# Score matmuls in PE tiles of 64 rows by 32 columns

## The chip, the cores and the metric

The kernel runs on one core of a Trainium2 chip. The metric is the device time of one execution in microseconds; lower is better. Three executions were timed before the change, and one more was recorded by the hardware profiler.

## What is computed

Three stages follow each other. The first is a linear attention with decay over 4 batches, 8 heads, 768 tokens and 48 features a head:

```python
for t in range(S):
    cur = np.einsum('bhd,bhe->bhde', u[None] * kt, vt)
    y[:, :, t] = np.einsum('bhd,bhde->bhe', rt, state + cur)
    state = w[None, :, :, None] * state + np.einsum('bhd,bhe->bhde', kt, vt)
```

The second and the third are `g(x @ w_in) @ w_out` over the 3072 tokens with 384 features and 2048 hidden units; the second has a leaky ReLU with a slope for each hidden unit, the third has `h * tanh(softplus(h))`.

## The kernel before, in words

**Work items.** The tokens are cut into 24 chunks of 128 tokens (a batch has six) and into 8 tiles of 384 tokens, three chunks each. The 8 heads of a chunk make four pairs. A unit is one pair of one chunk, so there are 96 units, numbered w = 4c + p. Head q of a pair (0 or 1) has its 48 features in partitions 64q to 64q+47, so that it takes one half of TensorE's rows.

**Scores by levels.** The 128x128 lower triangle of scores of a chunk is not computed at once, because the decay between two tokens must be split between a scaled key and a scaled query. It is cut into seven levels. Level l has m = 2^l: in every block of 2m tokens, the second m tokens (queries) look at the first m (keys). GpSimd scales the keys and queries of levels 1 to 6 (L272, L262); level 0 takes the rows as they came. `score` (from L993) writes for each level the products of all 128 keys with the 64 tokens that are queries at this level, head q into PSUM bank q, keys on partitions, at the columns `level_columns(l)`. What isn't needed of this is never read: ScalarE copies the blocks of the high levels (`copy_high`, L804), VectorE picks the low ones under a mask (`pick_scores`, L539). So keys of one half only meet queries of their half: two halves of 64 keys, each with 32 queries, two heads, four matmuls for each of levels 0 to 5; level 6 has the first 64 keys alone, against 64 queries, two matmuls. That is 26 matmuls (L1021) a unit. They are float32, and the profile shows each as two pairs of a weight load and a matmul: 52 pairs a unit. Keys are the stationary operand, queries the moving one.

**A unit on the engines.** ScalarE writes the diagonal of the scores (`fill_diagonal`, L792), waits for the unit's score matmuls, and copies the high levels (L804). VectorE then adds the chunk's sum into the running state (`advance_state`, L523), which waits for these copies, and picks the low levels (L539, five instructions). TensorE then runs `attend`: the state's part (L1038) and, after the picks, scores times values (L1043). Before the scores of a unit TensorE computes the chunk's sum of keys times values (L1005).

**Order on TensorE.** In the first tile units run alone (`first_tile`). Then `tile1` runs 16 steps for each tile, and in each step: the up projection of the tile before (`up`, L960, nine matmuls of 384 columns), `attend` of the unit of the last step, `score` of this step's unit, and the down projection of two steps back (`down`, L976, nine matmuls). Of 16 steps 12 have a unit. Meanwhile ScalarE has for each step the two ReLU parts (L841, L842) and the high part of the hidden values (L771), and VectorE the activation (L636) and their low part (L618), each in a fixed order with the unit's work between them. The third stage (`tile2`) has no units.

The lines that the change and the working touch: L1015 to L1021 in `score`, and the readers L804, L523 and L539.

Of the kernel before, what the change touches and what calls it, by code (L numbers as in the profile page):

```python
# [39 lines left out]
CHUNK = 128  # L40
CHUNKS = TOKENS // CHUNK
PAIRS = H // 2
HALF = 64
ROWS = HALF + D
LEVELS = CHUNK.bit_length() - 1
LOW = 5
# [23 lines left out]
def spread(ap, axis, n):  # L70

    wide = ap.unsqueeze(axis)
    return wide.broadcast_to([n if i == axis else k for i, k in enumerate(wide.shape)])


def build(nc, rk_t, rkv, decay, bonus, slope, weights, out):
# [4 lines left out]
    with ctx:  # L81
        def sb(name, shape, dt=F32):
            return ctx.enter_context(nc.sbuf_tensor(name, shape, dt))

        def sem(name):
# [21 lines left out]
                                                                l=LEVELS - 1)  # L107
# [19 lines left out]
        half = sb("half", [P, 1])  # L127
# [11 lines left out]
        hid2 = hid + [lev[:, i] for i in range(2)]  # L139
        U0 = (LEVELS - 1) * HALF  # L140


        rev_table = acc[0][:, 0:PAIRS * HALF].rearrange("p (a t) -> p a t", a=PAIRS)
        fwd_table = acc[2][:, 0:PAIRS * HALF].rearrange("p (a t) -> p a t", a=PAIRS)

# [57 lines left out]
        block = ctx.enter_context(nc.Block())  # L203
# [28 lines left out]
        def level_banks(rep, p):  # L232

            return hid_pair if rep == 0 and p % 2 else lev

        def level_columns(l):

            first = (l - 1) * HALF if l else U0 + D
            return slice(first, first + HALF)

# [14 lines left out]
        def scale_query_level(engine, par, x, l, early):  # L255

            pairs = slice(2 * x, 2 * x + 2)
            m = 1 << l
            src = rk_rows[0:ROWS, par, 0, pairs].rearrange("p a (i b m) -> p a i b m", b=2, m=m)[:, :, :, 1]
            dst = queries[0:ROWS, x, l - 1].rearrange("p (a i m) -> p a i m", a=2, m=m)  # L260
            table = fwd_table if early else power
            return engine.tensor_tensor(dst, src, spread(table[0:ROWS, pairs, 0:m], 2, CHUNK // (2 * m)), ALU.mult)  # L262


        def scale_key_level(engine, par, x, l, early):

            pairs = slice(2 * x, 2 * x + 2)
            m = 1 << l
            src = rk_rows[0:ROWS, par, 1, pairs].rearrange("p a (i b m) -> p a i b m", b=2, m=m)[:, :, :, 0]
            dst = keys[0:ROWS, x, l - 1].rearrange("p (a i b m) -> p a i b m", a=2, b=2, m=m)[:, :, :, 0]  # L270
            table = rev_table if early else power_rev[:, :, CHUNK - HALF:CHUNK]
            return engine.tensor_tensor(dst, src, spread(table[0:ROWS, pairs, HALF - m:HALF], 2,  # L272
                                                         CHUNK // (2 * m)), ALU.mult)
# [663 lines left out]
        def _(pe):  # L937
# [45 lines left out]
            def ready(c, w, p, rep):  # L983

                if rep == 0:
                    reached(pe, mask_done, w - 1)
                elif p == 0:
                    pe.wait_ge(mask_done, w)
                if p % 2 == 0:
                    pe.wait_ge(key_done, 2 * c + p // 2 + 1)  # L990
                    pe.wait_ge(q_done[p // 2], c + 1)

            def score(c, w, par, p, rep, ends):  # L993


                x = p // 2
                banks = level_banks(rep, p)
                if not ends:
                    ready(c, w, p, rep)
                    if p == 0:  # L1000
                        pe.wait_ge(kstate_done, c + 1)
                    for q in range(2):
                        rows = slice(HALF * q, HALF * (q + 1))
                        h = 2 * p + q
                        nc.tensor.matmul(banks[rows, 0, U0:U0 + D], k_state[:, p, rows],  # L1005
                                         rkv_tok[:, par, 2, D * h:D * (h + 1)], start=True, stop=True)

                for l in reversed(range(LEVELS)):
                    if l:
                        k = keys[:, x, l - 1].rearrange("p (a t) -> p a t", a=2)[:, p % 2]  # L1010
                        t = queries[:, x, l - 1].rearrange("p (a t) -> p a t", a=2)[:, p % 2]
                    else:
                        k = rk_rows[:, par, 1, p]
                        t = rk_rows[:, par, 0, p].rearrange("p (i b) -> p i b", b=2)[:, :, 1]
                    parts = 1 if l == LEVELS - 1 else 2  # L1015
                    for half in range(parts):
                        tokens = slice(HALF * half, HALF * (half + 1))
                        wanted = slice(HALF // parts * half, HALF // parts * (half + 1))
                        for q in range(2):
                            rows = slice(HALF * q, HALF * q + D)  # L1020
                            last = nc.tensor.matmul(banks[tokens, q, level_columns(l)][:, wanted], k[rows, tokens],  # L1021
                                                    t[rows, wanted], start=True, stop=True)
                last.then_inc(score_done, 1)
# [23 lines left out]
            def first_tile():  # L1047

                units = CHUNKS_PER_TILE * PAIRS
                pe.wait_ge(zero_act, 3)  # L1050
                for w in range(units):
                    c, p = divmod(w, PAIRS)
                    score(c, w, c % 2, p, 0, False)
                    if w > 0:
                        c, p = divmod(w - 1, PAIRS)
                        attend(c, w - 1, c % 2, p, 0, c == 0)
                c = CHUNKS_PER_TILE - 1
                attend(c, units - 1, c % 2, PAIRS - 1, 0, False)
                score(c + 1, units, (c + 1) % 2, 0, 1, False)

            def tile1(t, rep):
                odd = rep % 2
                for j in range(STEPS):
                    s = STEPS * (t - 1) + j
                    if rep > 1 or j >= 2:
                        pe.wait_ge(glo_done, s - 1)
                    now = unit_at(j) if rep < TILES and (rep < TILES - 1 or j + 1 < STEPS) else None
                    if now:
                        c = CHUNKS_PER_TILE * t + now[0]
                        unit = (c, 4 * c + now[1], (odd + now[0]) % 2, now[1], rep)  # L1070
                    ends = now and odd == 1 and now[0] == CHUNKS_PER_TILE - 1
                    if ends and now[1] == 0:
                        ready(unit[0], unit[1], 0, rep)
                    up(s, j, 1 - odd, j + 1 if rep == 1 else None, hid[j % 2],
                       per_chunk * CHUNKS_PER_TILE * t if j == 0 else None)
                    if ends and now[1] == 2:
                        ready(unit[0], unit[1], 2, rep)
                    u = unit_at(j - 1)
                    if rep < TILES and u:
                        c = CHUNKS_PER_TILE * t + u[0]  # L1080
                        attend(c, 4 * c + u[1], (odd + u[0]) % 2, u[1], rep, odd == 0 and u[0] == 0)
                    if now:
                        score(*unit, ends)
                    if rep > 1 or j >= LAG1:
                        down((t - 1) if j >= LAG1 else (t - 2), (j - LAG1) % STEPS, ghi_done, s - LAG1 + 1,
                             glo_done, s - LAG1 + 1)
# [81 lines left out]
```

## Time and profile before

| what | us |
|---|---|
| runs (three) | 1051.43, 1058.20, 1057.89 |
| median | 1057.89 |
| the profiled execution | 1052.23 |
| its span, first to last instruction | 1050.2 |
| first tile, units alone | about 0 to 75 |
| tiles with units in their steps | about 75 to 580 |
| the rest, without units | 580 to 1050 |

The span is 2 us shorter than the time of the same execution; a change of the span counts one for one. PE stands for matmuls, PEld for weight loads. Durations of matmuls are modelled and overlap, so that their starts tell more than their ends. A row of the windows view counts the instructions that touch a stretch, with their busy time as a union.

### The profile page before, as it was taken

What the parts mean: (1) busy time and instruction counts of PE and PEld (TensorE: products, weight loads), DVE (VectorE), ACT (ScalarE), POOL (GpSimd) and SP (SyncE); (2) the same over time, 40 slices, a digit from 0 to 9 for tenths busy, and PEclk for the clock granted to TensorE, in tenths of its full rate; (3) what the DMA queues carried; (4) which work ended last, traced back from release to release, by engine and by line L of the source; (5) the groups of instructions that cost most, each with busy time, mean ns of one, the idle gap of its engine ahead of it and who ended that gap; (6) DMA issues with size and microseconds to landing.
All of it is one profiled execution on the core that took longest, in us unless ns stands there. A gap on an engine that the chain in (4) does not pass through costs nothing.

```text
span 1050.2 us, 28000 instructions
## 1 busy us (share of the span) xinstructions
PE 1001.7 (95%) x10628; PEld 949.2 (90%) x10628; DVE 692.5 (66%) x1643; ACT 684.7 (65%) x1698; POOL 378.2 (36%) x674
## 2 busy tenths in 40 slices
PE   4668999999989999999999999999999999999998
PEld 3557889999889999899999999999999999999998
DVE  6458676656646655566566444877777777787875
ACT  6545655455544555555555567888888888888885
POOL 7556657656646655556563062000000000000000
PEclk9999999999999999999999999999999999999999
DMA  3223322112121221221120243100000000000000
GB/s 107 88 77 118 118 73 66 43 43 66 44 68 44 58 66 46 58 70 49 43 66 6 103 120 98 61 24 24 24 23 22 22 22 22 22 0 22 1 23 23
DMA packets 22036, 54.50 MB, mean 52 GB/s; under 512 B 4640, under 2 KB 9376, under 8 KB 21920
## 3 DMA queue, kind: packets, MB, share of 16 engines
q1 hardware_dynamic: 19472, 43.43, 14.0%
q10 hardware_dynamic: 2448, 9.49, 2.3%
q8 instruction: 78, 1.28, 0.5%
q14 instruction: 38, 0.31, 0.1%
HBM read 41.10 MB, written 9.44 MB: 48 GB/s over the span
## 4 chain that ended last, share of the span: by engine, by line
PE 80%; ACT 4%; DVE 4%; issue 2%; DMA 2%; SPq 0%; ACTq 0%; DVEq 0%
PE acc L976 36%; PE hid L960 25%; PE lev L960 8%; PE lev L1021 7%; PE tok L1038 2%; PE tok L1043 2%; DMA w_raw<-weights 2%; DVE scores L539 1%; ACT scratch L884 1%; ACT scratch L885 1%; PE lev L1005 1%; DVE scratch L687 1%; ACT scores L792 0%; DVE scratch L680 0%; ACT scores L804 0%
## 5 line engine op out<-in xcount | busy, mean ns | idle before, releaser
L960 PE MATMUL hid<-x_parts,w_hi 128*128 128x384 f32 x1152 | 326.6, 337 | 9.5 <-DMA x_parts<-y 5.6
L976 PE MATMUL acc<-g_hi,w_hi 128*128 128x384 f32 x768 | 269.8, 351 | 1.6 <-ACT result L781 1.6
L976 PE MATMUL acc<-g_hi,w_lo 128*128 128x384 f32 x768 | 257.7, 335 | 0.0
L960 PEld LDWEIGHTS hid<-x_parts,w_hi 128*128 128x128 f32 x1152 | 212.6, 189 | 10.4 <-issue 10.2
L960 PE MATMUL hid<-x_parts,w_lo 128*128 128x384 f32 x576 | 194.0, 337 | 0.0
L841 ACT ACTIVATE relu_neg<-hid 128x384 f32<-128x384 f32 x128 | 62.6, 489 | 200.2 <-PE hid L960 199.7
L976 PE MATMUL acc<-g_lo,w_hi 128*128 128x384 f32 x768 | 175.1, 335 | 0.0
L539 DVE COPY_PREDICATED scores<-mask,lev 128x128 f32<-128x128 int8 x444 | 158.9, 358 | 12.0 <-issue 0.2
L636 DVE SCALAR_TENSOR_TENSOR hid<-relu_neg,neg_slope,hid 128x384 f32<-128x384 f32 x128 | 79.6, 622 | 128.3 <-ACT hid L842 128.2
L976 PEld LDWEIGHTS acc<-g_hi,w_hi 128*128 128x128 f32 x768 | 144.2, 188 | 11.1 <-issue 3.9
L272 POOL TENSOR_TENSOR scratch<-rk_rows,power_rev 112x128 f32<-112x128 f32 x240 | 97.4, 441 | 153.7 <-PE lev L1021 153.7
L976 PEld LDWEIGHTS acc<-g_hi,w_lo 128*128 128x128 f32 x768 | 144.6, 188 | 0.0
L976 PEld LDWEIGHTS acc<-g_lo,w_hi 128*128 128x128 f32 x768 | 137.2, 188 | 0.6 <-DVE g_lo L705 0.6
L262 POOL TENSOR_TENSOR scratch<-rk_rows,power 112x128 f32<-112x128 f32 x282 | 117.8, 454 | 0.1
L960 PEld LDWEIGHTS hid<-x_parts,w_lo 128*128 128x128 f32 x576 | 109.2, 190 | 0.0
L960 PE MATMUL lev<-x_parts,w_hi 128*128 128x384 f32 x384 | 107.6, 334 | 0.0
L891 ACT ACTIVATE scratch<-scratch,three_halves 128x384 f32<-128x384 f32 x128 | 78.7, 615 | 41.3 <-DVE scratch L687 40.8
L693 DVE SCALAR_TENSOR_TENSOR scratch<-scratch 128x384 f32<-128x384 f32 x128 | 71.5, 558 | 40.1 <-ACT scratch L891 40.1
L1021 PE MATMUL lev<-scratch 48*64 48x32 f32 (+1 forms) x3960 | 84.8, 229 | 0.0
L680 DVE TENSOR_SCALAR scratch<-scratch 128x384 f32<-128x384 f32 x128 | 46.1, 360 | 55.6 <-ACT scratch L885 55.6
L1021 PEld LDWEIGHTS lev<-scratch 48*64 48x64 f32 x3960 | 74.7, 141 | 7.5 <-issue 3.2
L618 DVE TENSOR_TENSOR g_lo<-hid,g_hi 128x384 fp32r<-128x384 f32 x128 | 70.6, 552 | 14.5 <-ACT g_hi L771 14.5
(95 smaller groups left out, 1534.1 us busy)
## 6 DMA issues: line engine op xcount, KB each, us to landing
rkv_tok<-rkv SPq DMA_DIRECT2D x24, 576.0 KB, 3.9
w_raw<-weights SPq DMA_DIRECT2D x32, 384.0 KB, 3.1
rk_rows<-rk_t SPq DMA_DIRECT2D x48, 192.0 KB, 3.3
x_dram<-result ACTq DMA_DIRECT2D x8, 576.0 KB, 3.1
rkv_tok<-x_dram SPq DMA_DIRECT2D x8, 576.0 KB, 3.7
out<-result ACTq DMA_DIRECT2D x8, 576.0 KB, 2.8
x_parts<-y SPq DMA_DIRECT2D x141, 16.0 KB
bonus_tok<-bonus SPq DMA_DIRECT2D x1, 192.0 KB, 5.5
```

The lines of the kernel that those rows point to most:

```text
L262: return engine.tensor_tensor(dst, src, spread(table[0:ROWS, pairs, 0:m], 2, CHUNK // (2 * m)), ALU.mult)
L272: return engine.tensor_tensor(dst, src, spread(table[0:ROWS, pairs, HALF - m:HALF], 2, CHUNK // (2 * m)), ALU.mult)
L539: nc.vector.copy_predicated(dst, pick, src).then_inc(pick_done if l < low_levels(rep) - 1 else mask_done, 1)
L618: nc.vector.tensor_tensor(g_lo[:, j % RING], hid[j % 2][:, 0:TILE], g_hi[:, j % RING].bitcast(F32), ALU.subtract).then_inc(glo_done, 1)
L636: nc.vector.scalar_tensor_tensor(hid[j % 2][:, 0:TILE], relu_neg[:, j % 2], neg_slope[:, j:j + 1], hid[j % 2][:, 0:TILE], ALU.mult, ALU.ad ...
L680: nc.vector.tensor_scalar(seed[:, d], seed[:, d], SEED_B, SEED_A, ALU.mult, ALU.add).then_inc(seed_done, 1)
L693: nc.vector.scalar_tensor_tensor(root[:, d], eps[:, d], 0.75, seed[:, d], ALU.add, ALU.mult).then_inc(root_done, 1)
L841: nc.scalar.activation(relu_neg[:, j % 2], hid[j % 2][:, 0:TILE], ACT.Relu, scale=-1.0)
L891: nc.scalar.activation(eps[:, d], eps[:, d], ACT.Square, scale=-1.0, bias=three_halves[:]).then_inc(sq_done, 1)
L960: last = nc.tensor.matmul(to[:, 0:TILE], w[:, j, kt * P:(kt + 1) * P], x[:, par, kt], start=x is x_hi and w is w_hi and kt == 0, stop=x is ...
L976: last = nc.tensor.matmul(acc[d][:, 0:TILE], w[:, j, cols], g[:, j % RING], start=j == 0 and g is g_hi and w is w_hi, stop=j == STEPS - 1 ...
L1021: last = nc.tensor.matmul(banks[tokens, q, level_columns(l)][:, wanted], k[rows, tokens], t[rows, wanted], start=True, stop=True)
```

## The change

`score` cuts the keys into groups of 32 instead of 64. With `block = max(2m, 32)`, a group of keys whose tokens are no keys at this level (second half of a block of 64 or 128) is left out, and a group meets only the queries of its own block. Levels 0 to 4 get four groups of 32 keys with 16 queries each, level 5 two groups with 32 queries, level 6 two groups with 64 queries; each for two heads. The outputs start at partitions 0, 32, 64 and 96, so that the eight combinations of head and key group take eight places of 64 rows by 32 columns. What is read later is the same.

```diff
+QUARTER = 32
...
-                    parts = 1 if l == LEVELS - 1 else 2
-                    for half in range(parts):
-                        tokens = slice(HALF * half, HALF * (half + 1))
-                        wanted = slice(HALF // parts * half, HALF // parts * (half + 1))
+                    m = 1 << l
+                    block = max(2 * m, QUARTER)
+                    for first in range(0, CHUNK, QUARTER):
+                        if first % block >= m > QUARTER // 2:
+                            continue
+                        tokens = slice(first, first + QUARTER)
+                        begin = first // block * block // 2
+                        wanted = slice(begin, begin + block // 2)
                         for q in range(2):
                             rows = slice(HALF * q, HALF * q + D)
                             last = nc.tensor.matmul(banks[tokens, q, level_columns(l)][:, wanted], k[rows, tokens],
```

## Rows read from the trace of the kernel before

**Rows 1.** The page: TensorE's share, its slices, and the chain that ended last.
```profile
PE 1001.7 (95%) x10628; PEld 949.2 (90%) x10628; DVE 692.5 (66%) x1643; ACT 684.7 (65%) x1698; POOL 378.2 (36%) x674
...
PE   4668999999989999999999999999999999999998
...
PE 80%; ACT 4%; DVE 4%; issue 2%; DMA 2%; SPq 0%; ACTq 0%; DVEq 0%
```

**Rows 2.** The windows view of L1021 alone: busy time and instructions by stage.
```profile
0.00:75.00 75.00, 23.46 (x723) 21.71 (x726) 1.00 0.34 95
75.00:138.00 63.00, 9.99 (x522) 8.88 (x520) 0.97 0.35 105
138.00:580.00 442.00, 72.80 (x3772) 64.72 (x3765) 1.00 0.18 53
```

**Rows 3.** Windows, L1021: one unit's burst, from its first load to the next line's.
```profile
308.47:309.41 0.94, 0.94 (x52) 0.89 (x52) 1.00 0.00 0
...
26.07:27.71 1.64, 1.64 (x52) 1.57 (x52) 1.00 0.45 125
```

**Rows 4.** Windows of 10 ns, L1021: matmuls, then loads, that touch each.
```profile
308.46:308.47 0.01, 0.00 (x0) 0.00 (x0) 1.00 0.00 0
...
308.50:308.51 0.01, 0.01 (x4) 0.01 (x4) 1.00 0.00 0
308.51:308.52 0.01, 0.01 (x4) 0.01 (x4) 1.00 0.00 0
308.52:308.53 0.01, 0.01 (x4) 0.01 (x5) 1.00 0.00 0
...
308.98:308.99 0.01, 0.01 (x16) 0.01 (x8) 1.00 0.00 0
309.00:309.01 0.01, 0.01 (x16) 0.01 (x12) 1.00 0.00 0
...
309.06:309.07 0.01, 0.01 (x16) 0.01 (x12) 1.00 0.00 0
```

**Rows 5.** Timeline of the loads after a burst: start, us, what.
```profile
304.66 0.19 PEld L976 LDWEIGHTS acc<-g_hi,w_hi 128*128 128x128 f32 x1
304.77 0.19 PEld L976 LDWEIGHTS acc<-g_hi,w_lo 128*128 128x128 f32 x1
```

**Rows 6.** Timeline of one step with the first unit of a chunk.
```profile
344.95 0.77 PEld L1021 LDWEIGHTS lev<-scratch 48*64 48x64 f32 x43
...
345.61 0.68 ACT L792 ACTIVATE scores<-ident,diag 128x128 f32<-128x128 f32 x2
...
346.37 0.61 ACT L804 ACTIVATE scores<-lev 64x128 f32<-64x128 f32 x3
...
347.35 1.91 DVE L539 COPY_PREDICATED scores<-mask,lev 128x128 f32<-128x128 int8 x5
...
349.21 0.17 PEld L1038 LDWEIGHTS tok<-r_state,state 112*48 112x48 f32 x4 [0.25 <-issue]
...
349.37 0.24 PEld L1043 LDWEIGHTS tok<-scores,rkv_tok 128*48 128x48 f32 x4
```

**Rows 7.** Timeline: later units of a chunk, the step after it.
```profile
327.71 0.61 ACT L804 ACTIVATE scores<-lev 64x128 f32<-64x128 f32 x3 [0.45 <-PE lev L1021]
...
328.69 1.93 DVE L539 COPY_PREDICATED scores<-mask,lev 128x128 f32<-128x128 int8 x5
...
331.05 0.24 PEld L1043 LDWEIGHTS tok<-scores,rkv_tok 128*48 128x48 f32 x4
...
332.67 0.61 ACT L804 ACTIVATE scores<-lev 64x128 f32<-64x128 f32 x3 [0.18 <-PE lev L1021]
```

**Rows 8.** Waits of PE, PEld and POOL for others: us in total, times, longest.
```profile
POOL scratch L272 <- PE lev L1021: 153.7, 20, 13.8
...
PEld tok L1043 <- DVE scores L539: 18.2, 25, 2.5
...
PE tok L1043 <- DVE scores L539: 11.8, 13, 2.1
```

**Rows 9.** Timeline of two units of the first tile: TensorE alone.
```profile
26.07 1.39 PE L1021 MATMUL lev<-scratch 48*64 48x64 f32 x42
...
28.33 0.67 PE L1043 MATMUL tok<-scores,rkv_tok 128*48 128x128 f32 x4 [0.55 <-DVE scores L539]
```

## The prediction

> **What bounds the kernel now.** I read the page first: how busy each engine is, the span in 40 slices, and the chain of work that ended last. TensorE is busy 95% of the span, its slices stand at 9 tenths (once 8) from the fifth on, and 80% of the last chain is TensorE's [rows 1]. So in most of the kernel a microsecond less on TensorE is a microsecond less of time, if nothing else is late next. The windows view of the changed line by stage shows how much there is to win: 73 us of the 442 between 138 and 580 us, 10 before that, and 23 in the first tile, where TensorE is not the bound; the last 470 us have no scores [rows 2]. Then I looked at one unit closely. From its first load to the first load of the down projection behind it a burst takes 0.94 us for 52 pairs of load and matmul, in the first tile 1.64 us [rows 3].
>
> **What sets a burst's 0.94 us.** There are four places in use (two heads by two key halves). The 10 ns windows show the rhythm. At the start the loads touching a window go from none to four within 40 ns: the four places are filled one after another, though in program order nine other pairs stand between the first pair and the one that opens the fourth place. A fifth load comes 50 to 60 ns after the first. Later the number of loads swings between 8 and 12, and 12 comes back about 60 ns later: four loads start nearly together, then nothing starts, then four again [rows 4]. So the engine doesn't run out of instructions; each place takes some 58 ns a pass. A pass of levels 0 to 5 streams only 32 columns. Its 58 ns are then mostly those of the load of 64 columns, in time for the next pass only. For a size that isn't 64 columns there is one pair of rows: the first load of 128 columns after a burst is followed by the next after 0.11 us [rows 5]. 64 columns in 55 ns and 128 in 110 ns make a load's time proportional to its columns.
>
> The sum fits. The places of the first key half have 14 passes (2 for each of seven levels), so 14 x 58 = 0.81 us, and 0.13 us is left for filling and draining: 0.94 us.
>
> **The change part by part.** *Instructions.* Levels 0 to 4 now have 8 matmuls each, levels 5 and 6 have 4 each: 48 matmuls, 96 pairs a unit in place of 52. Over 96 units that is 4224 more pairs. *Columns.* The loads fall from 52 x 64 to 96 x 32 columns, about the same in sum (3328 to 3072), but spread over eight places. *The longest place.* The places of keys 0 to 31 still have 14 passes, the others 12 or 10. Level 6 streams 64 columns as before; its two passes stay at 58 ns each, as a stream of 64 columns is about as long as its load was (estimate from attend's 128 columns, which come in about 0.11 us apart). The twelve others load 32 columns: half of 55 ns, plus the 3 ns by which 58 is over 55, about 31 ns. Their stream (16 columns, or 32 at level 5) fits into that. 2 x 58 + 12 x 31 = 0.49 us, plus 0.13 us for filling and draining: 0.62 us. Saved: 0.32 us a unit; I take 0.31, since eight places need 7 ns each to be filled.
>
> *Bounds of a pass.* No row has a 32-column load or eight places. From above: all 58 ns are fixed or shared, and nothing is won (0 us). In the middle: half is fixed (the matmul of a pass starts some 28 ns after its load) and only the other 27 ns halve, so 45 ns a pass, 2 x 58 + 12 x 45 = 0.66, and 0.79 us a unit: 0.15 saved. From below: a pass of 25 ns would save 0.39. Below nothing: if the engine could not start pairs faster than it does now on average (0.94/52 = 18 ns, or 0.79/52 = 15 ns without filling and draining), a unit would take 96 x 15 ns + 0.15 = 1.6 us, 0.67 us more. I take 31 ns, since the two load sizes seen lie on one line and the fill of the places at 7 ns each shows faster starts than 15 ns.
>
> The Trainium skill, TensorEngine Tiling (Array Packing), section Performance Considerations, speaks against this change: each matmul costs about 60 cycles whatever its free size, so one should not take a tiling factor from a dimension that is already small. Here the moving side shrinks from 32 to 16 columns. At 2.4 GHz that is 25 ns, and counted over the whole engine 96 x 25 ns = 2.4 us a unit. The trace doesn't agree with it in that sense, as 52 x 25 ns = 1.3 us is more than the 0.94 us measured; counted for each place it is under the 31 ns above.
>
> **What of it reaches the end.** *Steps with a unit, 138 to 580 us* (72 units). The mask of a unit must be there when the next step's attend starts. In the later units of a chunk ScalarE's copies wait for the scores (idle 0.45 and 0.18 us before L804 [rows 7]), so an earlier burst brings the mask earlier too; the picks end at 330.62 and attend's load starts at 331.05, 0.43 us spare. These units keep nearly all of the 0.31 us. In the first unit of a chunk no attend stands before the scores, and L804 starts right when L792 is done (345.61 + 0.68 against 346.37), about 0.45 us after the burst's end: ScalarE is the limit, and an earlier burst changes nothing for the mask. The picks end at 349.26, L1043 starts at 349.37 [rows 6]. With 0.31 us less before it, TensorE would wait 0.2 us there. That is so in about 13 of the 18 chunks, 2.4 us in all. The first unit of each tile already waits for VectorE (the view of waits has 25 waits of L1043's loads for L539, 18 us in sum [rows 8]); I leave about 7 units out. (72 - 7) x 0.31 - 2.4 = 17.8 us.
>
> *75 to 138 us* (some 10 units): here ScalarE and VectorE also split weights and TensorE often waits for the masks. Half of 0.31 for each: 1.5 us.
>
> *First tile* (12 units). A unit's attend waits for the picks (0.55 us idle [rows 9]), and the next score burst stands behind it; so the chain runs score, copies, picks, attend and the score of two units later, and a shorter burst counts once in two units. Matmuls are slower here, 1.64 us a burst [rows 3]. In the same proportion the saving is 0.31 x 1.64/0.94 = 0.54 us; twelve times, halved, 3.2 us. As DMA waits and VectorE's own work hold some of these units, I take 2.2.
>
> *At nothing.* GpSimd waits for scores, not the other way about, with 154 us of such waits [rows 8], and takes earlier keys gladly. VectorE at 66% and ScalarE at 65% [rows 1] are no bound on average. The reads of the scores don't change. Fetching 8448 more instructions has room, as a step of 4.9 us now has some 160 of TensorE's and would have 250; if that cover failed, it would be the slower case below.
>
> The sum: 17.8 + 1.5 + 2.2 = 21.5 us. From the profiled 1052.2 us that gives 1030.7. This execution lies 5.7 us under the median of the runs, 1057.9, near the lowest; from the median it would be 1036. I say 1033.
>
> **The rivals.** *A: half of a pass is fixed* (45 ns). 0.15 us a unit: mask waits are then small, 70 x 0.15 + 0.8 + 1.1, about 12 us; 1043. For it: the matmul of a pass starts 28 ns after its load. Against: the 128-column load would then be 83 ns and not 110.
> *B: places in the same rows share the path of the loads.* Four places of 32 columns need as long as two of 64, a pass stays at 58 ns, 14 of them: 1053 to 1058, no change. For it: the sum of columns stays, and two places by 27 ns would also give 55 ns. Against: four loads start within 20 ns and their next ones also, with none late. The same result follows if the masks turn out to hold TensorE everywhere: then only the first tile gains.
> *C, slower: starts become the bound.* One mechanism: pairs reach the array no faster than the 15 ns that the burst now shows. It decides from 0.81/96 = 8.5 ns a pair on; at 15 ns 0.67 us more for each of 84 units, with a mask that is spare longer: 56 us, 1108. At 10 ns it is 0.15 us a unit, 13 us, 1068. For it: no row shows more than a few starts at under 15 ns. Against: the fill at 7 ns a matmul, where at least ten pairs were at hand. The rule of the skill named above would give this sign.
> *D: the change doesn't do what it says*, for instance because the same drain and fill come between the groups of 32 as come between lines: that would be C again, in the profile as gaps inside a burst.
>
> **How the numbers follow.** My forecast (31 ns a pass, 28 to 36) 0.53; A 0.17; B 0.13; C with D 0.17. A measurement of this kernel can tell about 1% (10 us) from no change. Faster by over 1%: the forecast and all of A but the part close to the line, 0.69. Within 1%: B and that part, 0.14. Slower by over 1%: 0.17. The likeliest case's own range is 1025 to 1041. The 8 in 10 range reaches over A to the upper end of B, 1060; only C lies outside. The lower end, 1023, is a pass of 25 ns (0.39 us a unit: 27 us) from the profiled execution.
>
> **What would show it.** Right: L1021 with 96 pairs a unit and a burst of 0.62 us from its first load to the down projection's; eight loads together in the 10 ns windows every 31 ns or so; new waits of L1043 for L539 of about 0.2 us in the first unit of a chunk; the steps of later units at 4.6 instead of 4.9 us; 580 to the end unchanged at 470 us. Wrong: bursts of 0.8 (A), 0.94 (B) or over 1 us (C), or short bursts with all of the gain in waits of L1043.

## The result, and the profile after

The changed kernel takes 1059.2 us (median of 20 runs, 1056.27 to 1061.2) against 1054.12 us of the kernel before (20 runs on the same chip, 1050.5 to 1058.2): a ratio of 1.0046, interval 1.0033 to 1.0058. It is half a per cent slower, small but clear of the noise, where 2% faster was forecast. By the bounds of the prediction it belongs to "within 1%". The profiled execution took 1057.9 us with a span of 1055.8 us, 5.6 us more than before.

The page after, the same three lines as [rows 1]:

```profile
PE 1003.7 (95%) x14852; PEld 953.1 (90%) x14852; DVE 691.3 (65%) x1643; ACT 687.1 (65%) x1698; POOL 379.0 (36%) x674
...
PE   4569899999989999999999999999999999999998
...
PE 84%; DVE 3%; ACT 3%; issue 2%; DMA 1%; SPq 1%; ACTq 0%; DVEq 0%
```

The 4224 additional pairs are there (14852 against 10628 matmuls), TensorE is as full as before, and its share of the last chain rose from 80 to 84%. The expected relief isn't there. Where it is missing shows in the windows of the changed line (now L1026): three stages, then one unit's burst in a step with tiles and one in the first tile, each from the first load to the first load behind it. They answer to [rows 2, 3].

```profile
0.00:75.00 75.00, 19.52 (x1344) 17.58 (x1344) 1.00 0.34 96
75.00:138.00 63.00, 10.94 (x960) 9.87 (x960) 0.95 0.36 106
138.00:583.00 445.00, 76.88 (x6872) 69.75 (x6872) 1.00 0.18 54
...
357.84:358.83 0.99, 0.99 (x96) 0.96 (x96) 1.00 0.00 0
...
31.30:32.56 1.26, 1.25 (x96) 1.22 (x96) 1.00 0.05 13
```

In the steps a burst takes 0.99 us and not 0.62 (before 0.94); in the first tile it did get shorter, 1.26 against 1.64 us.

**Inside a burst.** The windows view of the same unit. The first row holds the burst's beginning; then comes a window of 10 ns behind it; the last four windows all begin at 358.24 us and each is 0.1 us longer than the one before, so that the difference of their counts is what started in that 0.1 us.

```profile
357.84:358.08 0.24, 0.24 (x32) 0.24 (x33) 1.00 0.00 0
...
358.15:358.16 0.01, 0.01 (x23) 0.01 (x4) 1.00 0.00 0
...
358.24:358.34 0.10, 0.10 (x24) 0.10 (x20) 1.00 0.00 0
358.24:358.44 0.20, 0.20 (x36) 0.20 (x32) 1.00 0.00 0
358.24:358.54 0.30, 0.30 (x48) 0.30 (x44) 1.00 0.00 0
358.24:358.64 0.40, 0.40 (x60) 0.40 (x56) 1.00 0.00 0
```

The first 32 pairs are gone in 0.24 us, 7.5 ns a pair. Then hardly anything starts for 0.1 us: only four loads touch the window at 358.15. From 358.34 on exactly 12 loads and 12 matmuls start in each 0.1 us, one pair in 8.33 ns (float32 matmuls start two together every 16.7 ns). Whether that depends on what the places do, the experiments ask. So the burst is 0.24 us for 32 pairs, about 0.11 us of pause, 64 x 8.33 ns = 0.53 us, and 0.11 us from the last matmul's start to the next load: 0.99 us. In [rows 4], with four places, loads came in groups of four some 60 ns apart: there the places set the pace.

**Where the 5.6 us are.** The timeline of the loads at the start of four units, after and then before:

```profile
149.20 0.20 PEld L1026 LDWEIGHTS lev<-scratch 48*32 48x32 f32 x14
...
296.04 0.15 PEld L1026 LDWEIGHTS lev<-scratch 48*32 48x32 f32 x10
...
306.25 0.15 PEld L1026 LDWEIGHTS lev<-scratch 48*32 48x32 f32 x9
...
582.48 0.32 PEld L1026 LDWEIGHTS lev<-scratch 48*32 48x32 f32 x32 [0.18 <-issue]
```

```profile
149.31 0.16 PEld L1021 LDWEIGHTS lev<-scratch 48*64 48x64 f32 x4
...
294.38 0.14 PEld L1021 LDWEIGHTS lev<-scratch 48*64 48x64 f32 x2
...
303.69 0.18 PEld L1021 LDWEIGHTS lev<-scratch 48*64 48x64 f32 x2
...
577.11 0.22 PEld L1021 LDWEIGHTS lev<-scratch 48*64 48x64 f32 x8 [0.18 <-issue]
```

At unit 24 both kernels stand within 0.1 us of each other (149.20, 149.31): the first tile won nothing. From unit 24 to 48 the steps take 146.84 us against 145.07, from 49 to 95 276.23 against 273.42: 4.6 us more. The bursts alone explain this: the 70 of these two stretches, each from its first load to the next line's, take 70.5 us in sum against 65.5 before. The usual one grew by 0.055 us (3.9 us for 70), and eight of them last 1.10 to 1.18 us instead of 0.99. The step from unit 48 to 49 crosses the loop edge, where TensorE's program jumps back in its loop over the tiles; it grew from 9.31 to 10.21 us. After the last unit both need 473 us. The sum is 5.5 of the 5.6 us.

At that loop edge and in the first tile there is one thing more, in the timeline of the matmuls after:

```profile
28.32 0.73 PE L1026 MATMUL hid<-scratch 48*32 48x16 f32 x48
29.83 0.34 PE L1026 MATMUL hid<-rk_rows 48*32 48x16 f32 x16 [0.78 <-issue]
...
50.97 0.88 PE L1026 MATMUL lev<-scratch 48*32 48x64 f32 x49
53.17 0.38 PE L1026 MATMUL lev<-scratch 48*32 48x16 f32 x24 [1.31 <-issue]
...
302.63 0.68 PE L961 MATMUL hid<-x_parts,w_hi 128*128 128x384 f32 x1 [3.74 <-issue]
```

A burst stops in its middle, here with 0.8 and 1.3 us of idle time, and with no semaphore to wait for. From the start of one matmul to the next there are four such stops of 0.5 to 1.5 us in the first 60 us and one at 103.8 us; before, no burst there has one. The stops of the first tile eat what its shorter bursts win. Before the first matmul behind the loop edge TensorE is idle for 3.7 us, before the change for 2.9.

### The profile page after: what moved, and what is told of

Its sections match the earlier page's. It is cut to its first block, busy times and chain, and to the rows that moved or that the text cites. A ratio compares the mean times of both kernels' runs of the same rounds, so it can differ in the third digit from the quotient of the medians.

```text
span 1055.8 us, 36448 instructions
## 1 busy us (share of the span) xinstructions
PE 1003.7 (95%) x14852; PEld 953.1 (90%) x14852; DVE 691.3 (65%) x1643; ACT 687.1 (65%) x1698; POOL 379.0 (36%) x674
## 4 chain that ended last, share of the span: by engine, by line
PE 84%; DVE 3%; ACT 3%; issue 2%; DMA 1%; SPq 1%; ACTq 0%; DVEq 0%
PE acc L977 37%; PE hid L961 27%; PE lev L961 8%; PE lev L1026 7%; PE tok L1043 2%; PE tok L1048 2%; DVE scores L540 1%; DMA w_raw<-weights 1%; PE lev L1006 1%; ACT scratch L886 1%; DVE scratch L688 1%; ACT scratch L885 1%; SPq L283 0%; ACT scores L805 0%; DVE scratch L681 0%
## 5 line engine op out<-in xcount | busy, mean ns | idle before, releaser
L1026 PE MATMUL lev<-scratch 48*32 48x16 f32 (+2 forms) x7200 | 86.8, 196 | 1.7 <-issue 1.6
L1026 PEld LDWEIGHTS lev<-scratch 48*32 48x32 f32 x7200 | 77.6, 108 | 9.6 <-issue 5.2
```

## The experiments

One theory, S in the texts below, was set against the rivals: pairs are supplied to TensorE no faster than one in 8.33 ns as soon as a first stock of 32 is used up. It was read from the trace of the kernel after, and the runs below test it. It predicts by the number of pairs; B (shared path of the loads) predicts by columns. Of each kernel the row of windows is one unit's burst in a step with tiles, from the first load to the next line's. Where no number of runs is given, a time is that of one run; runs of the kernel before spread over 8 us, so that in these cases the bursts say more than the times.

**Half the columns in each load.** From the kernel after. Half of the keys are left out (each load takes the first 16 of its 32); the columns of the two highest levels are cleared beforehand.

```diff
-                        tokens = slice(first, first + QUARTER)
+                        tokens = slice(first, first + QUARTER // 2)
```

> The changed kernel, with each load cut from 32 keys to the first 16 of its group (half of the keys are left out of the scores; the 48 matmuls, their places and their queries stay). A burst of the changed kernel takes 0.99 us from its first load to the down projection's. Theory S (supply): after the first 30 pairs, pairs reach the array one per 8.33 ns whatever they hold, so the burst stays at 0.97 to 1.00 us. Rival B (places in the same rows share the path of the loads, a pass being bound by the columns loaded there): the burst falls to about 0.6 us.

Measured: 1059.21 us, beside 1059.07 of the kernel before, which is also the time beside the next three kernels.

```profile
355.56:356.51 0.95, 0.95 (x96) 0.92 (x96) 1.00 0.98 407
```

Halving all loads takes 0.04 us off a burst; B had said about 0.6 us. B is refuted: the columns of the loads don't set the pace. The burst is a little shorter than S had said (0.97): the first 32 pairs, which aren't bound by the supply, are gone 0.02 us sooner. In a single run the time shows no gain.

**32 moving columns instead of 16.** From the kernel after: at levels 0 to 4 a group of keys meets all 32 queries of its half, those of the other block included.

```diff
+                        if block == QUARTER:
+                            wanted = slice(first // HALF * QUARTER, first // HALF * QUARTER + QUARTER)
```

> The changed kernel, with 32 queries in place of 16 in each matmul of levels 0 to 4 (the other 16 products are never read). Theory S: the stream of a pass grows from about 13 to 27 ns, still under the 67 ns that a place has per pass (8 places x 8.33 ns), so the burst stays at 0.97 to 1.01 us. A theory in which places share the path of the moving operand: 40 matmuls x 2 passes x 13 ns more over two row halves, 0.5 us more.

Measured: 1061.08 us.

```profile
355.83:356.83 1.00, 1.00 (x96) 0.96 (x96) 1.00 0.91 364
```

Twice the moving columns cost 0.01 us a burst. What the change saved on the moving side was worth next to nothing.

**Fewer pairs, the same matmuls.** From the kernel after: scaled keys and queries of levels 1 to 6 as bfloat16, so that their matmuls are one pair and not two. There remain 48 matmuls, but 56 pairs. The scores are coarser by that.

```diff
-        keys = scratch[:, 0:k_size].rearrange(...)
+        keys = scratch[:, 0:k_size // 2].bitcast(BF16).rearrange(...)
```

> The changed kernel, with the scaled keys and queries of levels 1 to 6 kept as bfloat16 (coarser scores; level 0 stays float32). The 48 matmuls of the program stay, but 40 of them become one pair in place of two: 56 pairs. Tells what the supply counts. S by pairs (8.33 ns each): 56 x 8.33 + 0.19 = 0.66 us a burst. S by the program's matmuls (16.7 ns each): 48 x 16.7 + 0.19 = 0.99 us, no change. Rival B: under 0.6 us.

Measured: 1023.7 us. The burst, its first 32 pairs, the pause behind them (no load starts), and two windows that differ by 0.04 us:

```profile
358.36:358.93 0.57, 0.57 (x56) 0.52 (x56) 1.00 0.00 0
...
358.36:358.49 0.13, 0.13 (x32) 0.13 (x33) 1.00 0.00 0
...
358.57:358.58 0.01, 0.01 (x28) 0.00 (x1) 1.00 0.00 0
358.58:358.62 0.04, 0.04 (x27) 0.03 (x4) 1.00 0.00 0
358.58:358.66 0.08, 0.08 (x32) 0.07 (x8) 1.00 0.00 0
```

This is the clearest picture of S. Here the first 32 pairs take 0.13 us, 4 ns a pair; then again nothing starts for 0.1 us; and then loads come one by one: four have touched the first of the last two windows and eight the second, and the eight matmuls of one pair that are left start 8.3 ns apart from 358.59 to 358.65. Behind them the float32 matmuls of level 0 start two together every 16.7 ns again. The supply counts pairs, not matmuls and not columns. The burst is 0.09 us shorter than the 0.66 that S gave, all of it in the first 32 pairs (0.13 against 0.24 us), which S had taken to be as slow as those of float32.

**Four places of 32 columns, 52 pairs.** From the kernel before. Half of the keys are left out, as above.

```diff
-                        tokens = slice(HALF * half, HALF * (half + 1))
+                        tokens = slice(HALF * half, HALF * half + HALF // 2)
```

> The kernel before, with each load of 64 keys cut to its first 32 (the other half of the keys is left out): 26 matmuls, four places, half of the loaded columns. It measures what a pass of 32 columns costs where the supply doesn't bind. My forecast's 31 ns a pass: 2 x 58 + 12 x 31 ns + 0.13 = 0.62 us a burst, in place of 0.94. A pass of 45 ns (half of it fixed): 0.79 us. A pass that doesn't depend on its columns: 0.94 us. Theory S needs at least 26 x 16.7 + 0.1 = 0.53 us and so allows all three.

Measured: 1034.13 us.

```profile
366.35:367.01 0.66, 0.66 (x52) 0.62 (x52) 1.00 0.00 0
```

In the middle of this burst the matmuls of one place start at 366.51, 366.54, 366.57, 366.61, 366.64, 366.67 and 366.70 us, 31 to 32 ns apart: the 31 ns a pass of the forecast are right, and A with its 45 ns (0.79 us a burst) is not. Toward the end the supply shows, with 12 loads between 366.75 and 366.85 us, since four places at 31.5 ns would take one in 7.9 ns. That lies behind the 0.04 us over the expected 0.62. So four places of this size already use all of the supply.

**Fewer pairs in eight places, and in four.** From the kernel after and from the kernel before; levels 0 and 1 are left out in both.

```diff
-                for l in reversed(range(LEVELS)):
+                for l in reversed(range(2, LEVELS)):
```

> The changed kernel without the scores of levels 0 and 1: 32 matmuls, 64 pairs, in place of 96. Theory S (a pair per 8.33 ns once the queue's first 32 pairs are gone): 32 x 8.33 = 0.27 us less, a burst of 0.72 us in place of 0.99. Passes of 31.5 ns as the bound would take away 4 x 31.5 = 0.13 us (0.86).

> The kernel before without the scores of levels 0 and 1: 18 matmuls, 36 pairs in four places. The longest place loses 4 passes of 58 ns: 0.94 - 0.23 = 0.70 us a burst. Theory S, if the supply bound the kernel before too: 16 x 8.33 = 0.13 us less (0.80).

Measured: 1038.99 us in eight places, 1037.88 in four (beside 1052.41 of the kernel before). First the burst in eight places, then that in four:

```profile
369.57:370.29 0.72, 0.72 (x64) 0.69 (x64) 1.00 0.00 0
```

```profile
364.08:364.78 0.70, 0.70 (x36) 0.66 (x36) 1.00 0.82 151
```

In eight places 32 pairs fewer take 0.27 us off (0.99 to 0.72), 32 x 8.33 ns. In four places 16 pairs fewer take 0.24 us off (0.23 to the last matmul's start, four passes of 58 ns), as the passes of a place had said and the supply alone had not (16 x 8.33 = 0.13). So the two kernels are bound by different things that cost nearly the same.

**Loads trimmed to what is read.** From the kernel before: the keys behind the last one that is read at a level are left off, the pairs stay 52 in four places.

```diff
-                        tokens = slice(HALF * half, HALF * (half + 1))
+                        tokens = slice(HALF * half, HALF * half + (HALF // 2 + 1 if l == LEVELS - 2 else HALF - (1 << l) % HALF))
```

> The kernel before, in its four places and with its 26 matmuls, but a load ends at the last key that its level reads: 63, 62, 60, 56 and 48 columns at levels 0 to 4, 33 at level 5 (32 would make it another place size), 64 at level 6. What is read is the same. If a pass is bound by its load at about 0.83 ns a column, the longest place saves 2 x (1+2+4+8+16+31) x 0.83 = 0.10 us a burst, 0.84 in place of 0.94 us, some 7 us in all: ratio 0.993 to the kernel before. If only half of the load's time goes with its columns: 3 us. If a pass doesn't depend on its columns: no difference, ratio 1.000. Theory S sees no change in the number of matmuls (26), which stays under what the supply allows.

Measured: 1048.04 us (12 runs) against 1053.51 of the kernel before on that chip, ratio 0.9949, interval 0.993 to 0.9967. It is half a per cent faster than the kernel before, clear of the noise, while the kernel after was half a per cent slower. The burst, and then four of the forms of load, each with its busy time and the mean ns of one:

```profile
368.71:369.57 0.86, 0.86 (x52) 0.81 (x52) 1.00 0.94 150
```

```profile
L1021 PEld LDWEIGHTS lev<-scratch 48*33 48x33 f32 x720 | 24.6, 111 | 0.3 <-issue 0.3
...
L1021 PEld LDWEIGHTS lev<-scratch 48*62 48x62 f32 x720 | 21.8, 141 | 0.0
...
L1021 PEld LDWEIGHTS lev<-scratch 48*48 48x48 f32 x720 | 18.7, 125 | 0.0
...
L1021 PEld LDWEIGHTS lev<-scratch 48*64 48x64 f32 x360 | 18.3, 138 | 7.6 <-issue 3.4
```

With fewer columns in sum at the same number of pairs the burst falls by 0.08 us; of 84 x 0.08 = 6.7 us the medians show 5.5. I had expected 0.10 us. The rest is one of the two passes of level 5. In a place of the first key half the first load of 33 columns starts at 368.82 us and the next at 368.88, 58 ns later as with 64 columns before; the one after that comes 29 ns later, at 368.91. The first of them stands behind level 6's stream of 64 columns, which probably holds it. From level 4 on the loads of this place are 46, 52, 55, 56 and 58 ns apart, as their columns say.

**Two sizes of place in a unit.** From the kernel after: only levels 5 and 6 in groups of 32 keys, levels 0 to 4 in halves of 64. That is 56 pairs, four more than before.

```diff
-                    block = max(2 * m, QUARTER)
-                    for first in range(0, CHUNK, QUARTER):
+                    size = QUARTER if l >= LOW else HALF
+                    block = max(2 * m, size)
+                    for first in range(0, CHUNK, size):
```

> Levels 5 and 6 in groups of 32 keys as in the changed kernel (8 matmuls), levels 0 to 4 in halves of 64 keys as before (20 matmuls): 28 matmuls with one change of the place size between them. By the longest place: 2 x 58 + 2 x 31 + 10 x 58 ns + 0.13 = 0.89 us. If the array drains at a change of the place size inside a line as it does between lines (about 0.1 us from the last matmul to the next load), 0.99 us or more; if it doesn't, 0.89 us and some 3 us less in all. Theory S: 28 x 16.7 ns is no bound.

Measured: 1057.68 us (12 runs) against 1053.51, ratio 1.0044, interval 1.0027 to 1.006. The burst, windows:

```profile
376.46:377.47 1.01, 1.01 (x56) 0.93 (x56) 1.00 0.81 205
...
376.46:376.61 0.15, 0.15 (x14) 0.15 (x16) 1.00 0.26 61
...
376.73:376.74 0.01, 0.01 (x10) 0.00 (x0) 1.00 2.74 461
376.76:376.77 0.01, 0.01 (x10) 0.01 (x3) 1.00 0.00 0
```

The 16 loads of the two high levels are out within 0.15 us; the next load, the first of 64 columns, stands at 376.75 us, 0.15 us later, with none between (the window at 376.73). Then four places take 58 ns a pass. From the last matmul of the small places to that load it is 0.12 us; from the last matmul of a burst to the down projection's first load, where the size changes too, it is 0.15 us in the kernel before and 0.11 us after. So a change of the size inside a burst stops the loads for 0.15 us and makes it 0.12 us longer than the sum without a stop (0.89), more than the short passes give back. D, as written, supposed such gaps between the groups of one size; the kernel after has none.

**bfloat16 in four places.** From the kernel before, the same edit as in eight places: 26 matmuls, 30 pairs. It is the smallest number of pairs tried, and it has the coarser scores.

> The kernel before with the scaled keys and queries of levels 1 to 6 as bfloat16, as in e3_bf16 but in the four places: 22 matmuls of one pair and 4 of two, 30 pairs in all, which fit into the queue before the burst starts. A place has 8 passes. If a pass of bfloat16 takes 58 ns as in float32: 8 x 58 + 0.13 = 0.59 us a burst, as much as the 0.57 of e3_bf16. If the load of 64 columns is faster in bfloat16 (27 ns), about 0.4 us, and this beats the eight places.

Measured: 1019.71 us (4 runs) against 1052.41, ratio 0.9681, interval 0.9644 to 0.9718. The burst, and then the longest wait of the loads for another engine:

```profile
353.00:353.42 0.42, 0.42 (x30) 0.38 (x30) 1.00 0.89 143
```

```profile
PEld tok L1044 <- DVE scores L540: 33.4, 40, 4.2
```

The matmuls of one place start some 32 ns apart here, though each load has 64 columns: to load a column of bfloat16 takes at most about half as long as one of float32. A burst is 0.52 us shorter (0.42 against 0.94), 44 us for 84 units; the first tile gives 4 us more (the 13th unit starts at 58.2 us, before at 62.1), and 33 us reach the end. The rest is where the prediction had put it: the waits of attend's loads for the picks rose from 18.2 us in 25 places [rows 8] to 33.4 in 40.

**Halves in the first tile alone.** From the kernel after, to see what the stops there cost.

```diff
-                    block = max(2 * m, QUARTER)
-                    for first in range(0, CHUNK, QUARTER):
-                        if first % block >= m > QUARTER // 2:
+                    size = HALF if rep == 0 else QUARTER
+                    block = max(2 * m, size)
+                    for first in range(0, CHUNK, size):
+                        if first % block >= m > size // 2:
```

> The changed kernel, but with halves of 64 keys (26 matmuls) in the units of the first tile; the 84 others keep the groups of 32. In the changed kernel TensorE stands still in the middle of some bursts of the first tile (1.3 us at 51.8, 1.2 us at 56), with nothing to wait for. If these are stops of the instruction supply, owed to the longer run of instructions, no gap over 0.3 us is left inside a burst before 62 us here, and bursts there take 1.64 us again; later bursts stay at 0.99 us. In time: the shorter bursts of the first tile (1.26 us) and the stops about cancel in the changed kernel, so unit 12 starts within 1 us of its 62.1 us and the whole within 2 us of it, 1055 to 1061 us. If the gaps are something else, they stay.

Measured: 1061.3 us, beside 1055.72 of the kernel before. There is no stop inside a burst of the first 12 units any more, and the 13th unit starts at 61.6 us (after 62.1): the stops and the shorter bursts of the first tile do cancel. The total lies just above the expected 1055 to 1061 us, and the trace shows where: unit 24 starts at 151.98 us, 2.8 us later than in the kernel after (149.20), and from there to the end both need about 907 us. So the difference arose between 62 and 152 us and not in the first tile; what made it there isn't shown.

## Why the prediction was wrong

**What bounds the kernel: right.** TensorE's 95% did decide. In the steps from unit 24 on, 5.0 us more in the bursts came out as 4.6 us at the end. Four places of 32 columns, with bursts 0.28 us shorter, took 1034.13 us, 20 us under the median of the kernel before; the way from 0.31 us a burst to 21.5 us was of the right size, as far as one run tells.

**The cause of 0.94 us: right.** The kernel before is held by its places, 14 passes of 58 ns, mostly load. Two runs show it: without levels 0 and 1 a burst loses four passes and not 16 x 8.33 ns, and trimmed loads shorten it at the same number of pairs. For this kernel "so the engine doesn't run out of instructions" holds too.

**31 ns a pass: right.** Four places of 32 columns run at 31 to 32 ns. A (half of a pass fixed) and B (a shared path, so that halved loads gain nothing by themselves) are both refuted.

**The burst of 96 pairs: here it failed.** The sum 2 x 58 + 12 x 31 ns + 0.13 = 0.62 us has only the passes of the fullest place in it. It put the supply of pairs at nothing, because "the engine doesn't run out of instructions" with 52 pairs and because "the fill of the places at 7 ns each shows faster starts than 15 ns". Measured is 0.99 us: 0.24 for 32 pairs, 0.11 of pause, 0.53 for 64 pairs and 0.11 to the next load. The starts at 7 ns are real, but they are those of the first 32 pairs of a burst, which lay ready: 0.24 us for 32 pairs after, 0.13 us in bfloat16. Behind them the supply is 12 pairs in 0.1 us, whatever they contain. Twelve passes of 31 ns in eight places would need a pair every 4 ns, twice as fast as they are supplied. Four places of 31.5 ns already need 7.9. I took a rate from the first ten pairs and used it for 96. The rows that I had read could not show this: in a burst of 52 pairs held by its places the average, 15 ns a pair, is the places' rate, which is no bound of the supply from either side.

**C had the mechanism and the wrong price.** It said that pairs reach the array too slowly, from 8.5 ns a pair on slower than before. The measured 8.33 ns is almost that point, which is why the result is so near to no change; with the pause and the quick first 32 pairs it is 0.055 us on the bad side of it. I had priced C only at 10 and 15 ns, since 15 was what the burst showed, and put "no change" down to B. That the time lies in the range (1023 to 1060) is luck: the range reached so far up for B, which is refuted. Two ends were off as well, without weight for this: 27 us under the profiled execution is 1025 and not 1023, and 13 us over it 1065 and not 1068.

**Filling and draining.** 0.13 us was assumed. From the last matmul's start to the next load it is 0.11 us after (0.15 before), and the pause of about 0.1 us after the first 32 pairs was in no term.

**The first tile.** "2.2 us": the bursts did shrink (1.64 to 1.26 us), but the 13th unit starts at 62.1 us in both kernels, so nothing of it was kept. "Fetching 8448 more instructions has room" is the step in doubt. The profile's queues show 110 packets of instructions against 78 in all, and the view of DMA has 10 against 6 before 62 us; in the first tile the stops fall in bursts of 96 pairs alone. The kernels with halved loads and with 32 moving columns have five there, of up to 2.1 us, and no kernel with 64 pairs or fewer in its first tile has one. Short bursts aren't safe everywhere, though: behind the loop edge one burst stops for 0.6 us with four places of 32 columns and one for 0.4 us with trimmed loads, both of 52 pairs. That the stops, and the 0.9 us more at the loop edge, are waits for instructions to be fetched is a guess that no run tried, so their cause stays open.

**Waits for the masks.** The added waits didn't come, as no burst of the steps got shorter. The waits of attend's loads for the picks are 14.6 us in 20 places after, 18.2 us in 25 before [rows 8]. The mechanism itself was right, as the bfloat16 kernel shows.

The Trainium skill's rule, TensorEngine Tiling (Array Packing), section Performance Considerations, is that a tiling factor isn't to be taken from a dimension that is already small; it gives each matmul an overhead of some 60 cycles. The advice held here. The figure, taken over the whole engine, didn't: 60 cycles would be 25 ns, and the runs show one pair in 8.33 ns, at 16 moving columns and at 32. The Trainium skill, TensorE: Matmul & The Clock Gate, section Architectural detail: the array is 16× 32×32, not 1× 128×128, gives TensorE a queue of 64 instructions. The trace agrees: 32 pairs, which are 64 instructions, go before the pause, in both number formats.

## What to carry to other kernels

Ask of a burst of small matmuls which of two sums is the longer: the time of a pass (load and stream, by columns) times the passes of the fullest place, or the first 32 pairs, a pause of 0.1 us and 8.33 ns for each pair behind them. Splitting into more places shortens the first and, where it adds pairs, lengthens the second; here four places of 32 columns already reach the supply, so that more than four only cost. Once the two are equal, only fewer pairs (a format with one pair a matmul) or smaller loads at the same number of pairs still help.

A rate read from the beginning of a burst is the rate of what lay ready. Before using it for the whole, look whether any stretch of the trace keeps it up for more pairs than the 32 that lay ready here, and price the rival also just around its decision point and not only at its worst.

## What was unexpected of the hardware

- The supply: 12 pairs of load and matmul in 0.1 us, the same for 16 or 32 columns of weights, 16 or 32 moving columns, float32 or bfloat16. That is for the steps; in a burst of the first tile the same rate shows in stretches only. In float32 a matmul is two pairs, so 16.7 ns. All of this is seen by the profiler's records; no run here tells whether the recording itself has a part in the rate.
- After the first 32 pairs hardly anything starts for about 0.1 us, in the kernel after and in its bfloat16 form. What the queue does then isn't shown.
- A change of the size of the places inside a burst leaves 0.15 us without a load.
- A pass bound by its load goes by the columns (58 ns for 64 of float32, 52 for 56, 46 for 48), and one with 64 columns of bfloat16 takes 32 ns.
- Stops of 0.5 to 1.5 us with no semaphore inside bursts of 96 pairs, in the first tile above all; in the kernel after there is none behind 104 us.
